# Seven block products for the first MLP weight, the first step's standing between the uses of the last batch's end

## The reference, cut to what matters

```
attn_out = softmax(scale * pool2(q) @ k.T) @ v     # 4 x 8 heads, 576 pooled queries, 1152 keys, d 64
x = moe(attn_out)      # 4 causal attention experts, gated 2 of 4, [4, 576, 512]
h = x.T @ U @ V        # token mixing, rank 32
u = x + h.T            # 4 batches x 576 rows = 2304 rows of 512
ch = np.maximum(u @ w_ch1, 0.0) @ w_ch2            # 512 -> 2048 -> 512
return (u + ch).astype(np.float32)
```

## Time and profile before

| | us |
|---|---|
| median of the runs | 1193.37 |
| time of the profiled execution | 1195.76 |
| its span, first to last instruction | 1194.0 |
| TensorE busy in the span | 1135.8 (95%) |
| VectorE, ScalarE, GpSimd busy | 651.6, 543.9, 523.4 |
| instructions | 19539 |

### The profile page before, as it was taken

One profiled execution on the slowest core, in us unless ns is written; L12 is line 12 of the kernel. 1 busy time (PEld: TensorE's weight loads), 2 busy tenths in 40 slices (PEclk: granted clock), 3 DMA queues, 4 the chain that ended last, 5 costly groups with the idle time before them and its releaser, 6 DMA issues. The chain is left out here.

```text
span 1194.0 us, 19539 instructions
## 1 busy us (share of the span) xinstructions
PE 1135.8 (95%) x7232; PEld 951.8 (80%) x7232; DVE 651.6 (55%) x1370; ACT 543.9 (46%) x1131; POOL 523.4 (44%) x560
## 2 busy tenths in 40 slices
PE   6999999989999999997899999789999999999998
PEld 5777777777777778786777777489898989899896
DVE  5888877877888888866556565553121212122120
ACT  4666666556666666546565656633110201111110
POOL 6888899998888888734333333300000000000000
PEclk9999999999999999998999999999999999999999
DMA  8222111221111221002001010142100001010000
GB/s 205 61 60 61 56 46 51 60 60 46 51 55 60 60 60 41 22 27 115 2 1 41 1 45 24 40 146 62 53 1 27 27 1 53 0 53 0 27 1 27
DMA packets 47559, 54.56 MB, mean 46 GB/s; under 512 B 10992, under 2 KB 29424, under 8 KB 46960
## 3 DMA queue, kind: packets, MB, share of 16 engines
q1 hardware_dynamic: 46864, 53.12, 14.4%
q10 hardware_dynamic: 608, 0.30, 0.1%
HBM read 43.97 MB, written 9.44 MB: 45 GB/s over the span
## 5 line engine op out<-in xcount | busy, mean ns | idle before, releaser
L647 DVE TENSOR_REDUCE part_max<-psA 128x1 f32<-128x384 f32 x465 | 250.6, 556 | 59.4 <-PE psA L382 36.7
L576 ACT ACTIVATE pT<-psA 128x576 f32<-128x576 f32 x288 | 187.9, 653 | 165.5 <-PE psA L401 156.4
L270 POOL TENSOR_TENSOR pT<-pT 128x576 f32<-128x576 f32 x157 | 225.3, 1435 | 26.2 <-ACT pT L576 4.3
L382 PE MATMUL psA<-kT,qT 128*128 128x384 f32 x465 | 166.0, 379 | 11.5 <-DVE part_max L647 11.1
L415 PE MATMUL psA<-pT,v_raw 128*64 128x288 f32 x1152 | 153.8, 412 | 0.0
L1770 ACT ACTIVATE hid_hi<-psC 128x384 fp32r<-128x384 f32 x96 | 47.2, 492 | 198.7 <-PE psC L1695 198.6
L392 PE MATMUL psA<-qT,kT 128*128 128x288 f32 x576 | 132.2, 311 | 0.0
L1789 DVE SCALAR_TENSOR_TENSOR hid_lo<-psC,hid_hi 128x384 fp32r<-128x384 f32 x96 | 53.5, 558 | 137.9 <-ACT hid_hi L1770 137.9
L401 PE MATMUL psA<-qTm,kT 128*128 128x288 f32 x576 | 123.0, 295 | 0.5 <-ACT qTm L562 0.5
L415 PEld LDWEIGHTS psA<-pT,v_raw 128*64 128x64 f32 x1152 | 77.0, 136 | 53.2 <-issue 6.4
L1711 PE MATMUL psC<-w_hi,hid_hi 128*128 128x512 f32 x288 | 113.5, 394 | 0.0
(11 more groups left out here) (165 smaller groups left out, 1948.2 us busy)
## 6 DMA issues: line engine op xcount, KB each, us to landing
k_raw<-in_k SPq DMA_DIRECT2D x32, 288.0 KB, 2.9
v_raw<-in_v SPq DMA_DIRECT2D x32, 288.0 KB, 2.8
q_raw<-in_q SPq DMA_DIRECT2D x31, 256.0 KB, 3.3
w_raw<-in_moe_w_ch SPq DMA_DIRECT2D x1, 4096.0 KB, 12.3
u_rows<-x_all SPq DMA_DIRECT2D x16, 256.0 KB, 2.0
w_raw<-in_moe_w_ch SPq DMA_DIRECT2D x16, 256.0 KB, 2.6
u_first<-u_rows SPq DMA_DIRECT2D x3, 768.0 KB, 4.5
u_second<-u_rows SPq DMA_DIRECT2D x3, 768.0 KB, 4.7
```

The source lines that it names most:

```text
L270: nc.gpsimd.tensor_tensor(pT[:, KT, :], pT[:, KT, :], pT[:, j, :], ALU.add).then_inc(part_summed, 1)
L382: nc.tensor.matmul(maxes[n % 2][:, 0:PIECE], qT[h % 3][:, t * P:(t + 1) * P], kT[u][:, c * PIECE:(c + 1) * PIECE], start=True, stop=True). ...
L576: nc.scalar.activation(pT[:, j, :].rearrange("p (a c) -> p a c", a=2), scores[n % 2][:, :, 0:HALF], ACT.Exp, scale=0.5 * float(D) ** -0.5) ...
L647: nc.vector.tensor_reduce(part_max[u][:, t, c:c + 1], maxes[n % 2][:, 0:PIECE], AX.X, ALU.max).then_inc(max_freed[n % 2], 1)
```

## The change

**The first product.** A step of the new `mlp` is a pair of hidden tiles (row blocks 128 wide, one from each half of the hidden layer) for a group of 768 rows; there are 3 groups by 8 pairs, 24 steps. The 256 hidden columns by 768 rows of a step, with the inner 512 as two halves, are a 2 by 2 by 2 block product. It is formed from 7 block products in place of 8: four sums of weight blocks (`sum_w1`, GpSimd), four sums of input blocks (`sum_inputs`, once a group), seven products of 6 matmuls of 384 columns, and seven additions that put the quadrants together (`add`, VectorE, into SBUF). Products alternate between two PSUM banks; the six output tiles of a group stay in the other six banks over its eight steps. Between two products of step n stands a seventh of the 36 matmuls of step n-1's second product. `w1` and `w2` are loaded again, pair by pair, in every step, and split anew.

**The joint.** `mlp` is no block of its own any more and has no hardware loop. The first group's six input tiles are turned in uses `"ut"` of the last batch (`TURNS`), and the seven products of step 0 (`"first"`) stand between the uses of `END`. Output tiles of the last group's second half are saved one by one.

```diff
@@ experts
+    TURNS = {(2, 2): [("ut", 0), ("ut", 1)], (2, 3): [("ut", 2), ("ut", 3)],
+             (3, 0): [("ut", 4)], (3, 1): [("ut", 5)]}
+    W1_BEHIND = {("qk", 2, 1): 0, ("qk", E - 1, 0): 1}
+    W2_BEHIND = ("ut", 3)
-    END = [("p", E - 1, QT - 3), ("p", E - 1, QT - 2), ("pv", YC - 1, 0),
-           ("p", E - 1, QT - 1), ("pv", YC - 1, 1)] + [
-        ("wo", t) for t in range(QT)] + [("down",)] + [("u", t) for t in range(QT)]
+    END = [("p", E - 1, QT - 3), ("p", E - 1, QT - 2), ("pv", YC - 1, 0), ("first", 0),
+           ("p", E - 1, QT - 1), ("pv", YC - 1, 1), ("first", 1), ("wo", 0), ("wo", 1),
+           ("first", 2), ("wo", 2), ("first", 3), ("wo", 3), ("wo", 4), ("down",), ("first", 4),
+           ("first", 5), ("u", 0), ("u", 1), ("first", 6), ("u", 2), ("u", 3), ("u", 4)]
@@ gpsimd, at END[0] of the last batch (k_hi_again)
                     scale(batches * STEPS - 2)
                     scale(batches * STEPS - 1)
-                elif use == END[-1] and b == batches - 1:
-                    pool.wait_ge(w1_hi, KC)
-                    split_lo(nc.gpsimd, w1_s[1][:, KC - 1, :], w1_raw[:, KC - 1, :],
-                             w1_s[0][:, KC - 1, :]).then_inc(w1_lo, 1)
+                    hidden.lo_of_w2(pool, 0)
+                    hidden.sum_w1(pool, 1)
+                if b == batches - 1 and use == ("qk", 2, 0):
+                    hidden.sum_w1(pool, 0)
@@ tensor
+            first_product = hidden.steps.tensor(pe, first=True)
             over_segments(score, do)
+            wait_freed(batches - 1, [("u", t) for t in range(QT)])
+            hidden.steps.tensor(pe)
@@ vector
+            def end_work(use):
+                last = batches - 1
+                if use == END[0]:
...
+                    hidden.sum_inputs(dve, nc.vector, 0, 0)
+                    hidden.sum_inputs(dve, nc.vector, 0, 1)
+                    hidden.inputs_lo(dve, 0, 0)
+                elif use == ("pv", YC - 1, 0):
+                    hidden.inputs_lo(dve, 0, 1)
+                elif use == ("p", E - 1, QT - 1):
+                    hidden.inputs_lo(dve, 0, 2)
+                elif use == ("first", 1):
+                    hidden.sum_inputs(dve, nc.vector, 0, 2)
+                    first_step(("add", 0))
+                elif use == ("wo", 0):
+                    hidden.sum_inputs(dve, nc.vector, 0, 3)
+                    hidden.inputs_lo(dve, 0, 3)
+                elif use == ("wo", 1):
+                    hidden.inputs_lo(dve, 0, 4)
+                    first_step(("add", 1))
+                elif use == ("wo", 2):
+                    hidden.inputs_lo(dve, 0, 5)
+                elif use == ("wo", 3):
+                    first_step(("add", 2))
+                    hidden.inputs_lo(dve, 0, 6)
+                elif use == LAST_WO:
+                    hidden.lo_of_w1(dve, 1, 0)
+                    first_step(("hidden", 0))
+                elif use == ("down",):
+                    first_step(("add", 3))
+                    first_step(("add", 4))
+                elif use == ("u", 0):
+                    first_step(("hidden", 1))
+                    first_step(("add", 5))
+                elif use == ("u", 1):
+                    hidden.lo_of_w1(dve, 1, 1)
+                elif use == ("u", QT - 1):
+                    first_step(("hidden", 2))
+                    first_step(("add", 6))
+                    first_step(("hidden", 3))
@@ class Hidden
+    def load_w1(self, sp, n):
+        pair = n % self.PAIRS
+        if n > 0:
+            sp.wait_ge(self.w_lo_done, 2 * n)
+        for h, slot in ((1, 0), (0, 2)):
+            sp.dma_start(self.w[:, slot:slot + 2, :, :].rearrange("p s c n -> p (s c) n"),
+                         self.w1_v[:, h, pair, :, :]).then_inc(self.w_loaded, 16)
+    def sum_w1(self, pool, n):
...
+        pool.wait_ge(self.w_loaded, 32 * (n + 1))
+        ops.tensor_tensor(s1, a21, a22, ALU.add).then_inc(done, 1)
...          # s2 = s1 - a11, s3 = a11 - a21, s4 = a12 - s2, 256 elements each
@@ mlp
+        def gpsimd(pool):
+            for n in range(1, STEPS):
+                g, p = n // PAIRS, n % PAIRS
+                if n + 1 < STEPS:
+                    hidden.sum_w1(pool, n + 1)
+                hidden.lo_of_w2(pool, n)
+                if p == SUM_STEP and g + 1 < GROUPS:      # SUM_STEP = 6
+                    pool.wait_ge(x_copied, (g + 1) * TILES)
+                    pool.wait_ge(x_lo_done, 7 * (g + 1))
+                    for k in range(4):
+                        hidden.sum_inputs(pool, nc.gpsimd, g + 1, k)
@@ mlp, tensor
+            for n in range(1, STEPS):
+                g, p = n // PAIRS, n % PAIRS
+                for k in range(7):
+                    product(n, k)
+                    second(n - 1, todo, cuts[k], cuts[k + 1])
+                if g + 1 < GROUPS and p in TURN_STEPS:    # steps 3, 4, 5
+                    at = (g + 1) * TILES + 2 * TURN_STEPS.index(p)
+                    turn(at)
+                    turn(at + 1)
+            todo = seconds(STEPS - 1, tiles_first=True)
+            second(STEPS - 1, todo, 0, len(todo))
@@ mlp, scalar (order of a step)
+                hi_of_w2(n); copy_first(n); next_inputs(0); next_inputs(1); hidden_hi(n, 0)
+                next_inputs(2); hi_of_w1(n + 1, 0); next_inputs(3); hidden_hi(n, 1)
+                next_inputs(4); hi_of_w1(n + 1, 1); hidden_hi(n, 2); next_inputs(5)
+                hidden_hi(n, 3); next_inputs(6)            # then two copy_turned in steps 3, 4, 5
@@ mlp, vector (order of a step)
+                add(n, U2); next_inputs(0); add(n, C11); next_inputs(1); hidden_lo(n, 0)
+                add(n, U3); next_inputs(2); lo_of_w1(n + 1, 0); add(n, C22); add(n, U4)
+                next_inputs(3); hidden_lo(n, 1); add(n, C21); next_inputs(4)
+                lo_of_w1(n + 1, 1); hidden_lo(n, 2)       # rows(0, 3) here in a group's first step
+                add(n, C12); next_inputs(5); hidden_lo(n, 3); next_inputs(6)   # and rows(3, 6)
```

More of the change, by code:

```diff
@@ L945, in experts @@
                   for u in step_uses(e, i, s == 0, s == batches - 1)]
-    ORDER += [(batches - 1, u) for u in END]
+    ORDER += [(batches - 1, u) for u in END if u[0] != "first"]
     use_no = {bu: n for n, bu in enumerate(ORDER)}
     BANKS = 5
-    W1_BEHIND = {("pv", YC - 1, 1): (0, 1), ("wo", 1): (2,), ("wo", QT - 1): (3,)}
     room = ExitStack()
@@ L1194, in gpsimd @@
             over_segments(scale_pair, k_hi_again)
+            hidden.steps.gpsimd(pool)
         def tensor(pe, first=False):
@@ L1268, in product, with turn_u @@
                 mm.then_inc(filled, 1)
+            def turn_u(b, t):
+                out = claim(b, ("ut", t))
+                pe.wait_ge(hidden.u_loaded[0], 16)
+                for c in range(KC):
+                    mm = nc.tensor.transpose(out[:, c * P:(c + 1) * P],
+                                             hidden.u[0][:, t, c * P:(c + 1) * P], ident[:, :])
+                mm.then_inc(filled, 1)
             def turn_x(b, use):
@@ L1337, in do @@
                     turn_x(b, use)
+                elif kind == "ut":
+                    turn_u(b, use[1])
+                elif kind == "first":
+                    first_product(use[1])
                 elif kind == "qk":
@@ L1395, in copy_out @@
                         src[:, 0:(i + 1) * rows].rearrange("p (j c) -> p j c", c=rows), ACT.Copy)
+                elif use[0] == "ut":
+                    ins = nc.scalar.activation(
+                        hidden.xT[:, :, use[1] * P:(use[1] + 1) * P],
+                        src[:, :].rearrange("p (c n) -> p c n", c=KC), ACT.Copy)
                 elif use[0] == "vg":
@@ L1559, in do @@
                     rank_gates(b)
-                if b == batches - 1 and use == ("pv", YC - 1, 1):
-                    for c in range(KC - 1):
-                        dve.wait_ge(w1_hi, c + 1)
-                        split_lo(nc.vector, w1_s[1][:, c, :], w1_raw[:, c, :], w1_s[0][:, c, :]
-                                 ).then_inc(w1_lo, 1)
+                if b == batches - 1 and use in W1_BEHIND:
+                    hidden.lo_of_w1(dve, 0, W1_BEHIND[use])
+                if b == batches - 1 and use in END:
+                    end_work(use)
@@ new lines, in end_work @@
+            def end_work(use):
+                last = batches - 1
+                if use == END[0]:
+                    for t in range(hidden.TILES):
+                        dve.wait_ge(freed[bank(last, ("ut", t))], freed_value(last, ("ut", t)))
+                    hidden.sum_inputs(dve, nc.vector, 0, 0)
+                    hidden.sum_inputs(dve, nc.vector, 0, 1)
+                    hidden.inputs_lo(dve, 0, 0)
+                elif use == ("pv", YC - 1, 0):
+                    hidden.inputs_lo(dve, 0, 1)
+                elif use == ("p", E - 1, QT - 1):
+                    hidden.inputs_lo(dve, 0, 2)
+                elif use == ("first", 1):
```

(17 more changed lines are left out.)

662 lines of the change are left out of this document (458 added, 204 removed).

## The result

The changed kernel takes 1188.53 us in the median (1184.1 to 1194.37, 20 runs) against 1195.04 for the kernel before (1192.54 to 1196.88, 20 runs): ratio 0.9946, 95% interval 0.9936 to 0.9956. It is faster by 0.54%, some 6.5 us, where 26 were forecast. The profiled execution took 1186.41 with a span of 1184.6, 9.4 less than before.

The account below looks back on a forecast made before the run. TensorE alone was taken to bound the MLP, matmul count times price. Step 1's start 790.5 + matmuls and transposes 369.4 + stalls 4.7 + end 3.3 = span 1167.9; median 1167, range 1162 to 1174, with most of two rivals 1158 to 1180.

Parts of the forecast that it names:

- TensorE's count and the prices: MLP steps: 1008 matmuls of 384 columns instead of 1152, at 0.1734 us each, saving 25.0 us; a step takes 15.5.
- Nothing stalls: MLP steps: VectorE (8.3 us), ScalarE (5.4) and GpSimd (5.5) keep up within 15.5 us, least slack 2.1 us.
- Even 8 us would be in time: MLP weight loads into the single raw buffer: taken as 4 us, ends 2 to 8, all before ScalarE wants them.
- (a): Steps 3, 4, 5 of two groups: product 0 waits about 0.25 us for a turned tile's bank, six times, 1.5 us.
- (b): A group's first steps: the second product waits for VectorE's three row additions, 0.6 x 2 = 1.2 us.
- (c): Step 6 of two groups: VectorE's SBUF-only instructions wait for GpSimd's input sums, next product 0 late, 2 us.
- The joint: From the last batch's experts through `END`: experts 2.5 us longer, step 1 starts at about 790.5, ends 786 and 798.
- The end: From the last matmul to the span's end, last output tile saved alone: 3.3 us against 4.7 before.
- Rival 1: Joint and steps: no contention, all fits; step 1 starts at 786, stalls 1 us, median 1159; chance 0.14.
- Rival 2: Joint eats more than it gives: step 1 starts at 798, stalls 9 us, median 1179; chance 0.16.
- Rival 3: MLP steps stall as VectorE waits out GpSimd: about 2 us more a step, 46 in all, 1213; chance 0.05.
- Rival 4: MLP's dense stream: switching banks between small matmul groups costs 0.08 us each, 26 us, no change; chance 0.03.

Follow-up runs that it names:

- GpSimd quiet: Changed kernel with GpSimd's sums and low parts cut to 4 elements a partition from step 2 on; 1180.38 us, ratio 0.9880 to the kernel before.
- the experiments at the joint: Changed kernel with ScalarE copying step 1's product 0 first, step 2's `w1` loaded before the saved-rows wait, `u` rows a step later; 1183.24 us, ratio 0.9895.
- the finer cut: Changed kernel with each product cut into halves of 3 matmuls, 2 or 3 second-product matmuls behind each; 1192.7 us, ratio 0.9980.
- the queue's edit: Changed kernel with step 2's `w1` loaded before the wait for saved rows and the `u` rows a step later; 1187.75 us, ratio 0.9933.

## Why the prediction was right in direction and wrong in size

The measured median lies outside both ranges of the prediction. Two steps of it make 12.8 of the 16.7 us: a unit price (6.2) and the loads at the joint (6.6).

**TensorE's count and the prices: count right, price off when mixed.** No matmul was missed and the last 42 cost 0.2274. The step "a step is 42 x 0.1734 + 36 x 0.2275 = 15.5" failed: 15.74. The prices were those of long runs of one product. In the same rows the first chunk's product stood at 34.19 / 192 = 0.178, and I took the smaller price without asking what made that chunk dearer. Shown: it is for the most part not the changes (28, 14 and 8 a step), and it is not met waits and not the work of any one of VectorE, ScalarE, GpSimd or the loads. Nor is it the code outside a hardware loop as such: the last chunk of the kernel before stands outside its loop and has the low price.
```profile
1123.33 33.29 PE psC L1695 x192
```
The price also changes within one step. In step 9 of the changed kernel, product 0 and product 3 (start, us, what; the second row of each pair is the matmul behind the product):
```profile
931.10 0.87 PE L1999 MATMUL psC<-operand,w_hi_odd 128*128 128x384 f32 x4
...
932.16 0.40 PE L2028 MATMUL psC<-w_hi_even,hid_hi_even 128*128 128x512 f32 x1
...
937.90 0.86 PE L1999 MATMUL psC<-operand,w_hi_odd 128*128 128x384 f32 x4
...
938.94 0.39 PE L2028 MATMUL psC<-w_hi_even,hid_hi_even 128*128 128x512 f32 x1
```
Product 0 takes 1.06 us, product 3 takes 1.04, which is the old price. Between them the last matmul of a slice and the first of product 2 start late (at 935.39 and 935.69, 0.32 and 0.30 behind the one before, where 0.23 is usual), just when VectorE ends its additions to the rows. The products behind that short stop are at the old price, while step 10 is dear again. In step 17 the price of the products falls in the same way without a stop. What sets the price stays open. That several engines together do it was not tried.

**"Nothing stalls" in ordinary steps: right.** Steps 10 and 17 to 22 show no wait. VectorE is busy 8.58 to 9.27 us in the steps without additions to the rows (8.3 forecast), GpSimd 5.36 (5.5). The surplus of VectorE is the meeting with GpSimd that I had put at 0.6 us: the low part beside GpSimd takes 1.3 to 2.0 us in steps 17 to 22 and 0.56 with GpSimd quiet. The slack holds it.

**"Even 8 us would be in time": the step that failed for step 1.** I priced the loads by size and gave the first of them a whole step. Step 2's `w1` landed at 804.5, 9.6 us after its issue, behind 1536 KB of `u` rows (such loads took 8.2 us to land), and it had been issued late to begin with; step 1's `w2` can't go out before the rows are saved, and ScalarE waits for it ahead of the copy that frees a bank. 6.6 us where I had none, and the experiments at the joint give 4.9 of them back by order alone.

**(a) to (c), 4.7 forecast.** (a), turned tiles: 2.8 instead of 1.5 (8.1 less the 5.3 of the turns themselves). The idle time before each of the six products was the 0.25 us forecast, but a stop costs more than its idle time: before step 4 the eight transposes and the stop take 846.87 - 845.59 = 1.28 us in place of 8 x 0.11 = 0.88, and product 0 behind takes 1.17 in place of 1.05, so 0.5 a stop. (b), rows at a group's start: 0.16 us in step 9, the two late matmuls above, and nothing in step 17; the finer cut made more of that wait. (c), GpSimd and VectorE together: right as a mechanism, too small, and partly in the wrong place. With GpSimd quiet, steps 6, 7, 8 and 14, 15, 16 lose 4.2 us against 2.0 forecast, steps 1 and 2 another 3.2, the whole kernel 7.9. I had put all of it in step 6 and expected maxima above 1.5 us there alone; they are 2.40 in step 6, but also 2.42 in step 1, 3.15 in step 7 and 1.88 in step 18.

That agrees with the Trainium skill (SBUF — State Buffer, section "Who interferes with whom"), by which the two engines lock each other out where both inputs of VectorE's instruction lie in SBUF and GpSimd's reads SBUF. The pair in step 7 fits a wait for the end of the other's instruction: GpSimd's runs from 906.58 to 909.58, VectorE's starts at 907.24 and ends at 910.39, 0.81 behind, and takes 0.95 with GpSimd quiet. So the loss is the rest of a long GpSimd instruction, here 2.2 us, where I had counted on at most 1.84 beside one of the input sums.

**The joint: right within 1.3 us** (791.83 against 790.5), in part by luck. With the 2.5 us of the experts added, product 0 was due at 763.5 and came at 763.69, and the additions of VectorE do end the last wait, as forecast. But the experts slipped by 3.4 us and not 2.5 (VectorE's reciprocal at 759.69, before at 756.24), and `"wo"` started at 770.32 and not 768.7. The stretch of `"u"` made that good: it took 6.0 us and not 7.3. **The end: right** (3.15 against 3.3).

**The rivals.** Rival 1 is out (the steps stall, GpSimd costs 7.9 us). Rival 2 (1179) is out by its mechanism: step 1 did not start at 798. Rival 3 did not come: VectorE and GpSimd do meet in ordinary steps, but once a step and within the slack, not six times. Rival 4 (no change) lay nearest in time and was the right place to doubt, but the wrong cause: at most 0.007 us a change, not 0.08. What the range lacked was a case for loads at the joint, and a doubt about a unit price that multiplies 1794 matmuls: 1.7% of it is 6 us.

## What to carry to other kernels

Where work is moved across a border between two stages, walk each queue from the border on, DMA issues included: a load that "has a whole step" can stand behind a large one or behind a wait, and the engine that waits for it holds whatever is queued behind. Mend the orders of all queues together; mending one only moved the wait. And take a unit price from the stretch whose stream is most like the new one; where the same group shows two prices, the range must hold both.

## What the hardware showed that I had not expected

- A wait of 2.74 us on TensorE cost more than its length: the granted clock was 0.64 in the 4.8 us behind it, 1.00 behind two waits of 0.64 and 0.71 us that did the same work. Putting a product into that wait was worth 2.7 us. Behind the waits of 1.20 and 1.19 us before steps 8 and 16 the granted clock stayed at 1.00.
- The time of one kernel goes with its mean granted clock: 0.986 in runs of the changed kernel that took 1191.4 and 1194.4 us, 0.992 in the one that took 1184.1. In the stretch from 763 us on, in which TensorE works in short bursts, the changed kernel had 0.72 and the kernel with the queue's edit (its window below) 0.50, though nothing is edited before that point. There the first product of step 1 came 2.6 us later; how much of that is the clock was not separated:
```profile
763.00:768.00 5.00, 3.86 (x17) 2.97 (x17) 3.34 (x4) 2.31 (x4) 4.76 (x4) 0.50 0.00 0
```
- 59 more waits on values already reached, among 78 matmuls, cost TensorE nothing that a step of 15.77 us shows.
- Ordinary steps alternate between 15.71 and 15.77 us with the parity of the buffers in nearly every kernel here, whatever was made quiet. Why was not found.
